# Reordering the opening of a fused attention and two-MLP kernel: k and weight loads before a gate, two score steps ahead of the first layer block, one low part cut in thirds

## What is computed

```python
B, H, S, D = 8, 8, 576, 64          # pool = 8, so 72 pooled keys
k_p = k.reshape(B, H, Sp, pool, D).mean(axis=3)
v_p = v.reshape(B, H, Sp, pool, D).mean(axis=3)
scores = scale * np.matmul(q, k_p.transpose(0, 1, 3, 2))
scores = scores - np.max(scores, axis=-1, keepdims=True)
attn = np.exp(scores)
attn = attn / (np.sum(attn, axis=-1, keepdims=True) + 1e-09)
x = np.matmul(attn, v_p)             # then laid out as 4608 tokens x 512
h = np.maximum(np.maximum(x @ w1, x @ w2), x @ w3)      # 512 -> 768
x = h @ w_out                                           # 768 -> 512
h = x @ w_in                                            # 512 -> 2048
g = h - np.tanh(h)
out = g @ w_out2                                        # 2048 -> 512
```

## Time and profile before

| | |
|---|---|
| median of 3 runs | 1440.73 us (1439.23 to 1441.86) |
| the profiled execution's own time | 1439.83 us |
| its span, first to last instruction | 1438.0 us |
| TensorE matmul busy | 1424.2 us, 99% of the span |
| VectorE, ScalarE, GpSimd busy | 1006.7, 653.8, 96.4 us |
| first half tile, blocks 0 to 5 | 20.31 to about 54.6 us |
| DMA moved | 269.74 MB, mean 188 GB/s |

### The profile page before, as it was taken

One profiled execution on the slowest core, in us unless ns is written; L12 is line 12 of the kernel. 1 busy time (PEld: TensorE's weight loads), 2 busy tenths in 40 slices (PEclk: granted clock), 3 DMA queues, 4 the chain that ended last, 5 costly groups with the idle time before them and its releaser, 6 DMA issues.

```text
span 1438.0 us, 26270 instructions
## 1 busy us (share of the span) xinstructions
PE 1424.2 (99%) x10794; PEld 1236.1 (86%) x10794; DVE 1006.7 (70%) x1765; ACT 653.8 (45%) x1291; POOL 96.4 (7%) x140
## 2 busy tenths in 40 slices
PE   8899999999999999999999999999999999999998
PEld 7888888888888878788899999999999999999997
DVE  7786666665656555534887777777777777777777
ACT  3322222222222221223676665666666566665655
POOL 2302121212121100000000000000000000000000
PEclk9999999999999999999999999999999999999999
DMA  6544444443534211155977666676766667676551
GB/s 224 200 148 138 167 142 166 143 165 127 180 128 152 99 60 60 52 198 208 326 271 256 220 234 228 214 254 219 254 220 225 235 218 256 213 250 223 194 184 52
DMA packets 81335, 269.74 MB, mean 188 GB/s; under 512 B 7168, under 2 KB 21504, under 8 KB 69568
## 3 DMA queue, kind: packets, MB, share of 16 engines
q1 hardware_dynamic: 81216, 268.07, 54.0%
HBM read 210.89 MB, written 57.15 MB: 186 GB/s over the span
## 4 chain that ended last, share of the span: by engine, by line
PE 95%; DVE 2%; DMA 2%; ACT 0%; issue 0%; SPq 0%; DVEq 0%; ACTq 0%
PE psum L676 29%; PE psum L716 27%; PE psum L740 25%; PE psum L690 10%; PE psum L619 2%; PE psum L659 2%; DMA v_first<-in_v 0%; DMA w_raw<-in_w 0%; DMA w_mid_raw<-in_w_mid 0%; DVE probs L1059 0%; DMA k_first<-in_k 0%; DMA k_raw<-in_k 0%; PE psum L803 0%; DVE h L1091 0%; PE psum L698 0%
## 5 line engine op out<-in xcount | busy, mean ns | idle before, releaser
L676 PE MATMUL psum<-x,w 128*128 128x512 f32 (+1 forms) x2160 | 452.7, 370 | 5.8 <-ACT first_copy L844 3.1
L676 PEld LDWEIGHTS psum<-x,w 128*128 128x128 f32 x2160 | 375.7, 188 | 77.1 <-ACT first_copy L844 3.3
L716 PE MATMUL psum<-w_out_s,g 128*128 128x512 f32 x1668 | 404.7, 391 | 0.5 <-DVE g L1126 0.4
L716 PEld LDWEIGHTS psum<-w_out_s,g 128*128 128x128 f32 x1668 | 304.3, 188 | 58.8 <-DVE g L1126 1.4
L740 PEld LDWEIGHTS psum<-x_even,ring 128*128 128x128 f32 x1680 | 212.7, 191 | 6.5
L740 PE MATMUL psum<-x_even,ring 128*128 128x256 f32 x1680 | 215.0, 283 | 0.0
L1131 DVE SCALAR_TENSOR_TENSOR poly<-poly,u_sq 128x512 f32<-128x512 f32 x144 | 99.0, 688 | 141.1 <-ACT poly L896 141.1
L740 PEld LDWEIGHTS psum<-x_odd,ring 128*128 128x128 f32 x1344 | 170.0, 191 | 5.0
L740 PE MATMUL psum<-x_odd,ring 128*128 128x256 f32 x1344 | 171.9, 283 | 0.0
L852 ACT ACTIVATE h<-best 128x512 fp32r<-128x512 f32 (+1 forms) x60 | 35.4, 589 | 276.1 <-DVE best L1085 276.1
L690 PE MATMUL psum<-h,w_mid_s 128*128 128x512 f32 x648 | 152.3, 391 | 0.0
(11 more groups left out here) (82 smaller groups left out, 1085.8 us busy)
## 6 DMA issues: line engine op xcount, KB each, us to landing
ring<-w_scratch SPq DMA_DIRECT2D x72, 1024.0 KB, 5.1
ring<-w_scratch SPq DMA_DIRECT2D x72, 768.0 KB, 4.4
x_scratch<-x_stage SPq DMA_DIRECT2D x18, 1024.0 KB, 4.2
x_odd<-x_scratch SPq DMA_DIRECT2D x28, 512.0 KB, 5.5
x_even<-x_scratch SPq DMA_DIRECT2D x28, 512.0 KB, 5.5
x_scratch<-x_stage SPq DMA_DIRECT2D x18, 768.0 KB, 3.4
w_scratch<-w_stage SPq DMA_DIRECT2D x32, 384.0 KB, 2.6
v_raw<-in_v SPq DMA_DIRECT2D x21, 512.0 KB, 4.6
```

The source lines that it names most:

```text
L676: mm = pe.matmul(psum[:, bank, 0:hi - lo], w123[:, m, ws, n, c, :], x[:, xs, c, lo:hi], start=(c == 0 and ws + xs == 0), stop=(c == KC1 - ...
L716: mm = pe.matmul(psum[:, j, :], g_of(c)[:, gs, j * P:(j + 1) * P], w_out_s[:, row_of(c), ws, :], start=(m == 0 and gs + ws == 0), stop=(m ...
```

## The change

- SyncE issues the first two k pieces of batch 1 and piece 3 before the gate; behind the gate stands only piece 4. Piece 5 and the first two v pieces are issued at the entry `l1 0 3` of `ORDER`, pieces 6 and 7 at `l1 0 5` (before: `l1 0 4`).
- The score steps 2 and 3 on TensorE move from behind block 0 to between `attend 0` and block 0. The first attention product goes to banks 0 to 3 (`product_banks`), so that these scores need not wait for x.
- VectorE's shift becomes an entry of its own, `shift n`. The shift of step 2 comes right behind the low part of piece 1, that of step 3 behind block 0.
- The low part of piece 0 is made in thirds (`first_low 0, 1, 2`, one per weight matrix); two of them come behind `x_low 0`, and the three products of block 0 wait for one third each.
- The probabilities of step 0 are normalized by GpSimd, with the inverse kept in `row_max[:, 0]`, and transposed by VectorE after those of step 1.
- High parts: piece 3 moves from behind block 0 to ahead of it, piece 5 from behind block 2 to behind block 3, pieces 6 and 7 further back. Six warming matmuls instead of nine stand ahead of `attend 0`.

```diff
-LOW_ON_DVE = [p for p in PIECES if p not in LOW_ON_POOL]
+LOW_ON_DVE = [p for p in PIECES if p not in LOW_ON_POOL and p != ("w123", 0)]
...
-        ("warm", 14), ("score", 0), ("score", 1), ("exp", 0), ("exp", 1), ("warm", 14), ("pool_v",), ("warm", 9), ("norm", 0), ("turn", 0),
-        ("high", 0), ("norm", 1), ("turn", 1), ("low", 0), ("attend", 0), ("high", 1), ("low", 1), ("high", 2)]
+        ("warm", 14), ("score", 0), ("score", 1), ("shift", 0), ("shift", 1), ("exp", 0), ("exp", 1), ("warm", 14), ("pool_v",), ("warm", 6), ("norm", 0),
+        ("high", 0), ("norm", 1), ("turn", 1), ("turn", 0), ("first_low", 0), ("attend", 0), ("score", 2), ("score", 3),
+        ("first_low", 1), ("first_low", 2), ("high", 1), ("low", 1), ("high", 2), ("high", 3), ("shift", 2), ("exp", 2)]
...
-    after_l1 = [[("high", 3), ("score", 2), ("score", 3), ("norm", 2), ("turn", 2)], [("high", 4), ("norm", 3)],
-                [("high", 5), ("turn", 3)], [], [("attend", 1)], [("high", 6)]]
+    after_l1 = [[("shift", 3), ("norm", 2), ("turn", 2)], [("high", 4), ("norm", 3)],
+                [("turn", 3)], [("high", 5)], [("attend", 1)], []]
...
-            after_l1[1].append(("high", 7))
+            after_l1[0].append(("high", 6))
+            after_l1[2].append(("high", 7))
...
+        def product_banks(n):
+
+            return 0 if n == 0 else 4
...
-            load_piece(3)
-
-            wait_filled(sp, ("l1", 0, 1, 0, HALF), NW - 1)
             for p in range(2):
                 load_k(1, p)
+            load_piece(3)
+
+            wait_filled(sp, ("l1", 0, 1, 0, HALF), NW - 1)
             load_piece(4)
-            load_piece(5)
-            for p in range(2):
-                load_v(1, p)
 
             for entry in ORDER:
-                if entry == ("l1", 0, 4, 0, HALF):
+                if entry == ("l1", 0, 3, 0, HALF):
+                    load_piece(5)
+                    for p in range(2):
+                        load_v(1, p)
+                if entry == ("l1", 0, 5, 0, HALF):
...
+            pool.wait_ge(softmax_step, 3)
+            nc.gpsimd.tensor_tensor(probs[:, 0, :, 0:KEYS], probs[:, 0, :, 0:KEYS],
+                                    first_inv.unsqueeze(2).to_broadcast([P, GROUPS * 2, KEYS]), ALU.mult)\
+                .then_inc(first_normalized, 1)
...
+                    if t == 0 and lo == 0 and m == 0:
+                        pe.wait_ge(first_low, n + 1)
...
+            def first_piece_low(n):
+
+                _, raw, hi, lo = piece(0)
+                dve.wait_ge(piece_hi, 1)
+                nc.vector.tensor_tensor(lo[:, n], raw[:, n], as_f32(hi[:, n]), ALU.subtract).then_inc(first_low, 1)
```

More of the change, by code:

```diff
@@ L115, in then @@
             o.append(e)
-            if e[0] == "score" and e[1] != 3:
-                o.append(("exp", e[1]))
+            if e[0] == "score":
+                o.extend([("shift", e[1]), ("exp", e[1])])
             if e[0] == "score" and e[1] in LAST_STEP[:-2]:
@@ L192 @@
 L1_NUMBER = {e: i for i, e in enumerate(e for e in ORDER if e[0] == "l1")}
-for _kind, _count in (("score", STEPS), ("exp", STEPS), ("norm", STEPS), ("turn", STEPS), ("attend", len(ATTENDS)), ("step", EARLY)):
-    assert [e[1] for e in ORDER if e[0] == _kind] == list(range(_count))
+for _kind, _count in (("score", STEPS), ("shift", STEPS), ("exp", STEPS), ("norm", STEPS), ("turn", STEPS), ("attend", len(ATTENDS)), ("step", EARLY)):
+    assert sorted(e[1] for e in ORDER if e[0] == _kind) == list(range(_count))
 assert [e[1] for e in ORDER if e[0] == "high"] == list(range(len(PIECES) - len(LATE)))
@@ L300, in as_f32 @@
             return ap.bitcast(F32)
+        first_inv = row_max[:, 0]
         probs_zero = sem("probs_zero")
@@ L317, in fused_attention_mlps @@
         softmax_step = sem("softmax_step")
+        first_normalized = sem("first_normalized")
         shifted = sem("shifted")
@@ L341, in fused_attention_mlps @@
         low_by_pool = sem("low_by_pool")
+        first_low = sem("first_low")
         low_by_dve = sem("low_by_dve")
@@ L381, in wait_filled @@
             return bank
+        def product_banks(n):
+            return 0 if n == 0 else 4
         def x_parts(n):
             lo, hi = ATTENDS[n]
-            return [(psum[:, 4 + pr, 0:hi - lo], slice(lo % TB, lo % TB + hi - lo), PAIRS * n + pr + 1)
+            return [(psum[:, product_banks(n) + pr, 0:hi - lo], slice(lo % TB, lo % TB + hi - lo), PAIRS * n + pr + 1)
                     for pr in range(PAIRS)]
@@ L474, in _ @@
             load_q(3)
+            for p in range(2):
+                load_k(1, p)
             load_piece(3)
             wait_filled(sp, ("l1", 0, 1, 0, HALF), NW - 1)
-            for p in range(2):
-                load_k(1, p)
             load_piece(4)
-            load_piece(5)
-            for p in range(2):
-                load_v(1, p)
             for entry in ORDER:
-                if entry == ("l1", 0, 4, 0, HALF):
+                if entry == ("l1", 0, 3, 0, HALF):
+                    load_piece(5)
+                    for p in range(2):
+                        load_v(1, p)
+                if entry == ("l1", 0, 5, 0, HALF):
                     for i in range(MC1, MC1 + 2):
@@ L612, in score @@
                     pe.wait_ge(shifted, n - 1)
+                if product_of(n) >= 2:
                     wait_x(pe, product_of(n) - 1)
@@ L649, in attend @@
                     pe.wait_ge(v_reduced, 3 * batches_of(lo, hi)[-1][2])
-                pe.wait_ge(shifted, hi // P)
-                wait_x(pe, n - 1)
+                if n > 0:
+                    pe.wait_ge(shifted, hi // P)
+                if n > 1:
+                    wait_x(pe, n - 1)
                 first = lo - lo % TB
@@ L658, in attend @@
                                 rows = slice(pr * BLK, pr * BLK + keys)
-                                mm = pe.matmul(psum[odd * D:(odd + 1) * D, 4 + pr, start - lo:stop - lo],
+                                mm = pe.matmul(psum[odd * D:(odd + 1) * D, product_banks(n) + pr, start - lo:stop - lo],
                                                v_pooled[rows, b % 2, c, odd, :],
@@ L667, in layer1 @@
                 _, t, m, lo, hi = entry
-                if t == 0 and lo == 0:
+                if t == 0 and lo == 0 and m > 0:
                     wait_piece(pe, "w123", m)
                 for n in range(NW):
+                    if t == 0 and lo == 0 and m == 0:
+                        pe.wait_ge(first_low, n + 1)
                     bank = open_bank(entry, n)
@@ L1216, in _ @@
                     piece_low(entry[1])
-                if entry[0] == "score":
+                if entry[0] == "first_low":
+                    first_piece_low(entry[1])
+                if entry[0] == "shift":
                     row_shift(entry[1])
```

20 lines of the change are left out of this document (13 added, 7 removed).

## The result

| | before | changed |
|---|---|---|
| median of 6 runs each | 1440.53 us | 1450.55 us (1449.21 to 1452.68) |
| ratio, with its 95% interval | | 1.0074 [1.0061, 1.0087] |
| profiled execution, its span | 1439.8, 1438.0 | 1450.6, 1448.6 |
| start of block 5 | 50.12 | 59.02 |
| start of score 4 | 58.94 | 70.54 |

The change makes the kernel 0.74% slower, some 10 us. The direction and the place are those of the forecast, but its 1448 was 2.6 us too low by the median and 3.4 us by the ratio. The result is at the upper end of the forecast's range of 1443 to 1451: the median of 1450.55 lies just inside it, and the ratio, taken on the 1440.7 from which the forecast was reckoned, gives 1440.7 x 1.0074 = 1451.4, just outside (1449.5 to 1453.3 by its interval).

A forecast was written before the change was run, and what follows sets the result against it. TensorE, busy 1424.2 us or 99% of the span, was taken as the bound. Block 5 starting 6.1 us later plus 1.4 for the clock gave +7.5 on 1439.8, hence 1447.3, about 1448 by the median; range 1443 to 1451.

The forecast's parts named there:

- both steps turned: Opening: probabilities of steps 0 and 1 both transposed by 17.4 us, instead of 17.43; bounds 17.0 and 17.4.
- GpSimd's multiplication: Opening: GpSimd's new multiplication of 576 elements, from about 12.8 us, would cost 1.37 to 1.54 us.
- piece 5 issued: SyncE's queue: piece 5's load, behind two k loads waiting for VectorE's reductions, issued at 44.3 us, 12 us later than before.
- its landing: Piece 5's load takes 6.3 us, as piece 4's did, landing at 50.6; bounds 4.1 and 8.4 us.
- idle ahead of it: TensorE, free at 47.35 us, idles 8.8 us for piece 5; block 5 starts at 56.2, 6.1 us later than before.
- clock: After the idle time ahead of block 5, TensorE restarts slower, costing 1.4 us; bounds 0 and 2.8.
- later: Behind this stretch, with pieces 6 and 7 issued near 57.5 us, other waits may go or grow: taken as 0.
- The 3.11 us wait: TensorE's wait inside block 3, before its second product, for ScalarE's first copy of block 2; forecast to go.
- The signs named ahead: Profile signs: piece 5 issued at 44 to 45 us, ScalarE idle 8 or more, TensorE waiting 7 to 10, longer matmuls.
- Rival 2: Block 5: not slower, if piece 5 lands by 44.6 us; 2.8 us won, 1438 us (1436.5 to 1443). Chance 0.10.
- the opening: Up to block 0: scores 2 and 3 take 1.66 us, covering the 1.04 us wait for x; block 0 at 20.6.
- VectorE's small step: Step 1's scalar step at 13.5 us, beside GpSimd's multiplication, ends only when that does, shifting step 1 by 0.7 us.

The follow-up runs named there:

- e1: Changed kernel with piece 5 loaded right behind piece 4 at the gate again, its high part left behind block 3: 1443.12 us, ratio 1.0016.
- e2: e1 with the high part of piece 5 also back behind block 2: 1439.72 us, ratio 0.9997.
- e3: Kernel before, with only piece 5's load and two v loads moved to the entry of block 3, as in the change: 1450.97 us, ratio 1.0068.
- e12: Changed kernel with scores 2 and 3 back behind block 0, all else as changed: 1449.02 us, ratio 1.0056.
- e4: Changed kernel with 38 warming products, read by nobody, in front of block 5: 1450.45 us, ratio 1.0066.
- e8: e2 with step 3's q load ahead of pieces 1 and 2, no gate, high parts 4 and 5 one place forward: 1438.75 us, ratio 0.9985.
- e9: e8 with scores 2 and 3 back behind block 0: 1437.34 us, ratio 0.9976.
- e10: e8 with only score 3 back behind block 0, score 2 left ahead of it: 1438.73 us, ratio 0.9985.
- e11: e8 with six warming products, read by nothing, ahead of score 2: 1439.76 us, ratio 0.9991.
- e7: Changed kernel with step 3's q load ahead of pieces 1 and 2 and 38 warming products before block 5: 1449.64 us, ratio 1.0059.

## Why the prediction was right in its direction and too low in its size

| step of the forecast | forecast | measured |
|---|---|---|
| both steps turned | 17.4 | 16.84 |
| GpSimd's multiplication | 1.37 to 1.54 | 1.15 |
| block 0 starts | 20.6 | 23.14 |
| piece 4 issued, landed | 30.5, 35.3 | 32.0, 36.6 |
| first copy of block 2 | 36.8 | 38.04 |
| block 4, then attend 1 until | 41.0, 47.35 | 42.22, 48.65 |
| piece 5 issued | 44.3 | 45.49 |
| its landing | 6.3 | 8.0 |
| high and low part of it | 5.5 | 5.5 |
| block 5 starts | 56.2 | 59.02 |
| idle ahead of it | 8.8 | 10.37 |
| clock | +1.4 | +2.7 |
| later | 0 | -1.0 |

**Right.** The 3.11 us wait goes and 0.67 are left, block 2's first copy comes earlier, and none of it is kept, since piece 5 stands behind two k loads that wait for VectorE. The signs named ahead are there in kind, though three of the numbers are just outside: piece 5 issued at 45.49 (44 to 45 was named), ScalarE idle 7.10 us for it (8 or more), the wait that GpSimd ends 10.37 us long (7 to 10), and longer matmuls after it. e1, e2 and e3 show that this is the cause and not only the place. Rival 2 asked for piece 5 in memory by 44.6; it was issued only after that.

Three terms of the sum were too small, in order of time 1.2, 1.7 and 1.3 us.

**The first term that failed: the opening.** "They cover the wait for x", the forecast says of the two scores, and has them follow the attention product in 1.66 us. A wait inside them it puts at nothing, without a reason. They took 1.77 us of products and 2.92 us of waiting, and block 0 came 2.5 us late. Between block 0 and the gate 0.9 us came back (9.8 us forecast, 8.9 measured: high part 3 came at 24.80 as forecast, but as TensorE was late by then, the 0.7 us of waiting for it fell away), which leaves 1.5 us at the gate and 1.2 at piece 5's issue. By e12 the moved scores are worth 1.7 us at block 5's start. Nothing in the rows named showed a wait for instructions. The page of before lists instruction packets on a queue of their own, but I took no row of it and did not count instructions.

**Second: the landing, 8.0 for 6.3 us.** The row of piece 4 was taken for its neighbours; it was the fastest of the six in the earlier trace rows, whose median was 8.4. The loads beside it were k and v, 288 and 512 KB each, and a queue 95 to 101% busy from 50 to 54 us. The fit of the Trainium skill ("DMA: Bandwidth & Descriptors", "Anatomy of one DMA"), made for GpSimd-issued transfers, gave an estimate of 3.8 us, further away than my row; the trace does not bear it out here, where SyncE issues and other loads share the engines.

**Third: the clock, 2.7 for 1.4 us.** The figure was taken from the kernel's start, from two groups of 28 warming products that both ran while the clock read full; here the clock read 0.50, and the products are longer ones. The bound of 2.8 held. e4 shows it to be the clock: with the idle time filled, the 72 matmuls take 8.90 us.

The opening (1.2 at the issue) and the landing (1.7) give the 2.8 us at block 5's start, but for rounding; with the clock (1.3) and 1.0 regained later the sum is 3.1 us, and the span is 1448.6 - 1438.0 = 10.6 us longer, where 7.5 were forecast. The stated range, too, ended lower than its own terms: the forecast's bounds for the landing (+8.2) and the clock (2.8) give 1440.7 + 11.0 = 1451.7, above 1451.

**VectorE's small step** beside GpSimd's multiplication took 0.61 us where it takes 0.17, and ended at 13.93, when the multiplication did (12.76 + 1.15 = 13.91). That is what the forecast said of it; only the multiplication was shorter than forecast. It cost nothing: both steps were turned at 16.84, and the warming products ended at 17.11.

## What to carry to other kernels

A load moved behind another engine's progress costs its whole latency once that progress comes last: ask, for each load moved on an in-order queue, what the loads ahead of it on that queue wait for. Here the place of piece 5's load decided 8 to 10 us (e1, e3), and of the kernels tried those without the gate (e8, e9) have the lowest times. Long runs of very short matmuls are no free cover: count the instructions, not only their time, and look for "issue" waits near the instruction packets in the DMA view, above all where the data queue is full.

## What the runs showed of the hardware that was not expected

- TensorE can stop for want of instructions. Its instructions come in packets of 16 KB, 254 products and weight loads to each by the totals, and where the next packet is late it waits: 2.92 us in the changed kernel, e1 and e4 to e8 (the same to 0.01 us), 1.66 in e2. Moving instructions moves the wait (e10, e11), and with 36 long products between the short runs it stands one packet's load further on (e9) or nowhere (e12). It ends 2.2 to 2.6 us after the packet's start. That start comes 0.8 to 1.2 us after TensorE has reached instruction 698 with the data queue empty or emptying, and 3.5 to 3.8 us after with it full.
- The clock's fall is not a matter of the last wait's length alone. After 3.11 us it held (before), after 3.16 us it fell (e1). After one and the same wait of 2.92 us it held in the profiles of the changed kernel and e1 (1.00 from 24 to 26 us) and fell in those of e4 to e8. A half-clock stretch in the opening cost 1.2 to 2.0 us (the 120 matmuls took 15.87 to 16.66 us in e4 to e7 for 14.65), and one behind 10.37 us of idle time 2.70.
- A single GpSimd multiplication of 576 elements a partition took 1.15 us, less than its subtraction of 512 (3.90 / 3 = 1.30).
- A VectorE step that meets a running GpSimd instruction can end when that one ends: 13.93 and 13.91 in the changed kernel, 31.33 and 31.30 in the one before. VectorE's row sum beside the same multiplication (12.59 to 13.29) kept its 0.70 us.
